# An expert matrix of the slots fetched earlier, in eight blocks of unused rows, and the combine weights turned ahead of the slots' fold

## What is computed

```python
def _moe2_ref(x, phi, w1, w2) -> np.ndarray:
    ...
    logits = x @ phi
    d = logits - logits.max(0, keepdims=True)
    d = np.exp(d)
    d /= d.sum(0, keepdims=True) + 1e-09
    slot_input = d.T @ x
    ...
    for e in range(E):
        h = np.maximum(slot_input[e] @ w1[e], 0.0)
        slot_out[e] = h @ w2[e]
    slot_out = slot_out.reshape(n_slots, D)
    c = logits - logits.max(1, keepdims=True)
    c = np.exp(c)
    c /= c.sum(1, keepdims=True) + 1e-09
    return (c @ slot_out).astype(np.float32)
```

## Time and profile before

| | us |
|---|---|
| median of 3 runs | 384.02 |
| lowest and highest of them | 383.75, 384.81 |
| profiled execution, its own time | 383.24 |
| span of the profiled execution | 381.3 |

### The profile page before, as it was taken

One profiled execution on the slowest core, in us unless ns is written; L12 is line 12 of the kernel. 1 busy time (PEld: TensorE's weight loads), 2 busy tenths in 40 slices (PEclk: granted clock), 3 DMA queues, 4 the chain that ended last, 5 costly groups with the idle time before them and its releaser, 6 DMA issues.

```text
span 381.3 us, 14796 instructions
## 1 busy us (share of the span) xinstructions
PE 352.3 (92%) x5876; PEld 270.6 (71%) x5876; DVE 281.1 (74%) x561; ACT 220.8 (58%) x679; POOL 115.7 (30%) x179
## 2 busy tenths in 40 slices
PE   7699899998999999989999999999999999999780
PEld 7487777777777788666777777777777777664260
DVE  7999999999999744695676777767767767630272
ACT  3777788787888774234656565565656566401051
POOL 3443322334222350064233333222333331651000
PEclk9989999999999999989999999999999999999967
DMA  8987655667657997003085599494949679699539
GB/s 306 412 328 253 257 204 206 238 261 256 234 199 217 402 409 300 21 13 124 22 305 233 189 338 373 170 408 135 391 155 366 213 268 375 229 353 382 194 136 359
DMA packets 31235, 97.58 MB, mean 256 GB/s; under 512 B 3998, under 2 KB 14346, under 8 KB 29658
## 3 DMA queue, kind: packets, MB, share of 16 engines
q1 hardware_dynamic: 29402, 93.81, 66.2%
q0 software_dynamic: 1792, 3.17, 2.7%
HBM read 85.53 MB, written 11.45 MB: 254 GB/s over the span
## 4 chain that ended last, share of the span: by engine, by line
PE 48%; DMA 8%; DVE 8%; issue 1%; ACT 1%; DVEq 0%; SPq 0%; POOLq 0%
PE a_bank L750 19%; PE y_bank L759 18%; DMA combs<-free_rows,put_i 5%; DMA x_all<-combs 2%; PE a_bank L615 2%; PE a_bank L810 1%; PE y_bank L576 1%; PE y_bank L571 1%; DVE x_all L1517 1%; PE a_bank L954 1%; PE ktok_bank L623 1%; PE sums_bank L623 1%; PE y_bank L583 1%; DVE batch_t L1328 1%; DVE free_rows L1501 1%
## 5 line engine op out<-in xcount | busy, mean ns | idle before, releaser
L759 PE MATMUL y_bank<-w_sb,work 128*32 128x192 f32 x1664 | 78.6, 326 | 0.4 <-ACT work L1103 0.4
L750 PE MATMUL a_bank<-w_sb,work 128*32 128x256 f32 x1248 | 77.9, 382 | 0.1
L759 PEld LDWEIGHTS y_bank<-w_sb,work 128*32 128x32 f32 x1664 | 65.3, 110 | 8.2 <-DVE work L1367 0.8
L1553 POOL TENSOR_SCALAR_AFFINE_SELECT a_sb<-a_sb 128x512 f32<-128x512 f32 x48 | 43.2, 911 | 87.3 <-ACT a_sb L988 87.3
L750 PEld LDWEIGHTS a_bank<-w_sb,work 128*32 128x32 f32 x1248 | 42.3, 109 | 25.7 <-issue 13.2
L1076 ACT ACTIVATE work<-work 32x96 f32<-32x96 f32 x108 | 30.4, 282 | 41.4 <-PE a_bank L750 39.1
L998 ACT ACTIVATE bonus_v<-v_sb,bonus 128x48 f32<-128x48 f32 x192 | 45.1, 321 | 14.0 <-DVE x_all L1231 13.9
L1411 DVE TENSOR_TENSOR ys<-work 32x192 f32<-32x192 f32 x104 | 36.3, 349 | 9.9 <-ACT work L1103 9.2
L1367 DVE STREAM_TRANSPOSE work<-hid 128x256 f32<-128x256 f32 x53 | 23.6, 445 | 25.3 <-PE y_bank L759 23.3
L550 PE MATMUL a_bank<-r_in,k_in 64*128 64x128 f32 x384 | 31.1, 297 | 0.1
L550 PEld LDWEIGHTS a_bank<-r_in,k_in 64*128 64x128 f32 x384 | 24.9, 194 | 6.3 <-issue 5.3
(11 more groups left out here) (310 smaller groups left out, 580.0 us busy)
## 6 DMA issues: line engine op xcount, KB each, us to landing
w_sb<-in_moe_w SPq DMA_DIRECT2D x20, 1536.0 KB, 8.2
e_sb<-in_moe_w SPq DMA_DIRECT2D x9, 1536.0 KB, 11.8
wrk_sb<-in_wrk SPq DMA_DIRECT2D x16, 768.0 KB, 7.3
wrk_sb<-in_wrk SPq DMA_DIRECT2D x15, 780.0 KB
v_sb<-in_vt SPq DMA_DIRECT2D x16, 288.0 KB, 2.8
tokens<-x_all SPq DMA_DIRECT2D x4, 1152.0 KB, 22.1
x_all<-in_moe_w SPq DMA_DIRECT2D x3, 1536.0 KB, 9.2
out<-x_all SPq DMA_DIRECT2D x12, 384.0 KB, 3.9
```

The lines of the kernel that those rows point to most:

```text
L750: last = nc.tensor.matmul(out[SUB * g:SUB * (g + 1), 0:FB], x[:, kk, :], w1_sb[j][:, kk, FB * g:FB * (g + 1)], start=(kk == 0), stop=(kk = ...
L759: last = nc.tensor.matmul(bank[4][SUB * g:SUB * (g + 1), 0:YW], h_t[:, SUB * k:SUB * (k + 1)], w2_sb[j][:, k, d:d + YW], start=(b == 0), s ...
L1553: nc.gpsimd.affine_select(out=x, in_=x, compare_op=ALU.is_gt, fill=0.0, base=0, pattern=[[0, 2], [0, 2], [1, C]], channel_multiplier=-1).t ...
```

## The change

It has four parts. First, e2[4] no longer takes blocks 0 to 7 of `x_all` but the eight blocks 14, 15, 16, 25, 26, 27, 28 and 0, in three transfers of 3, 4 and 1 blocks, which SyncE issues right behind e1[5], after `stage_ready` 1. They lie in rows that the 13 groups don't use. Second, e1[7] moves to blocks 1 to 8 and is issued at `slot_parts_full` 2. Third, since `dispatch` still reads the blocks that are being filled, TensorE waits within it: for the first three blocks ahead of group 13, and for all of e2[4] ahead of group 24. The table `combs[3]` is gathered into `disp` and no longer into blocks 25 and 26. Fourth, at the end TensorE turns the combine weights ahead of the fold, ScalarE copies them ahead of its half of `slot_rows`, and VectorE adds the last table ahead of `parts` and makes the norms ahead of its half of `slot_rows`. Two products of the identity that nobody reads follow the fold.

```diff
-                     for t in (logit_t[:, 0:NB, :], weigh_t[:, 0:NB, :], x_all[:, TILES - 3:TILES - 1, :])]
+                     for t in (logit_t[:, 0:NB, :], weigh_t[:, 0:NB, :])] + [disp[:, 0:NT, :]]
...
-        LAST_GROUPS = LAST_PLACE // DM - 2
+        BLOCKS = [14, 15, 16, 25, 26, 27, 28, 0]
+        LAST_GROUPS = BLOCKS[0] - 1
...
-                 7: matrix(x_place[:, WIDE:2 * WIDE], DK, F)}
-        late2 = {4: matrix(x_place[:, 0:WIDE], FK, DM)}
+                 7: matrix(x_place[:, DM:DM + WIDE], DK, F)}
+        late2 = {}
...
+        def e2_rows(e, k):
+            return x_all[:, BLOCKS[k], :] if e == 4 else e2_place(e)[:, k, :]
...
+        def load_e2_blocks(eng, k0, k1, landed):
+
+            eng.dma_start(x_all[:, BLOCKS[k0]:BLOCKS[k0] + k1 - k0, :],
+                          e2[4].rearrange("(k p) d -> p k d", p=P)[:, k0:k1, :]).then_inc(landed, 16)
...
             load_e1(sp, 5)
+            sp.wait_ge(ld_e2[0], 16)
+            sp.wait_ge(stage_ready, 1)
+            load_e2_blocks(sp, 0, 3, ld_e1[5 % EH])
+            load_e2_blocks(sp, 3, 7, ld_e2[0])
+            load_e2_blocks(sp, 7, 8, ld_e2[0])
             sp.wait_ge(slot_parts_full, 2)
-            load_e2(sp, 4)
-            sp.wait_ge(slot_parts_full, 3)
             load_e1(sp, 7)
...
-            dispatch(B1, 4 * BATCH, B1, MAX_GROUPS, x_sorted, bank[1])
+            dispatch(B1, LAST_GROUPS, B1, MAX_GROUPS, x_sorted, bank[1])
             pe.wait_ge(ld_e1[5 % EH], last_landed)
+            dispatch(LAST_GROUPS, 4 * BATCH, B1, MAX_GROUPS, x_sorted, bank[1])
             pe.wait_ge(disp_ready, 5)
-            dispatch(4 * BATCH, MAX_GROUPS, B1, MAX_GROUPS, x_sorted, bank[1])
+            dispatch(4 * BATCH, MAX_GROUPS - 2, B1, MAX_GROUPS, x_sorted, bank[1])
+            pe.wait_ge(ld_e2[0], last_landed)
+            dispatch(MAX_GROUPS - 2, MAX_GROUPS, B1, MAX_GROUPS, x_sorted, bank[1])
...
-            pe.wait_ge(parts_ready, 2)
-            nc.tensor.matmul(bank[3][:, 0:DM // 2], all_parts, parts[:, 0:DM // 2], start=True, stop=True).then_inc(fold_done, 1)
-            nc.tensor.matmul(bank[1][:, 0:DM // 2], all_parts, parts[:, DM // 2:DM], start=True, stop=True).then_inc(fold_done, 1)
             pe.wait_ge(combs_added, 3)
             turn(exps, comb_transposed, 0, 4, bank[6])
             pe.wait_ge(combs_added, 4)
             turn(exps, comb_transposed, 4, NB, bank[7])
+            pe.wait_ge(parts_ready, 2)
+            nc.tensor.matmul(bank[3][:, 0:DM // 2], all_parts, parts[:, 0:DM // 2], start=True, stop=True).then_inc(fold_done, 1)
+            nc.tensor.matmul(bank[1][:, 0:DM // 2], all_parts, parts[:, DM // 2:DM], start=True, stop=True).then_inc(fold_done, 1)
+            idle_products(2, bank[4][:, 0:P])
...
-            dve.wait_ge(slot_back_done, E)
-            V.tensor_scalar(parts[:, 0:DM], bank[2][:, 0:DM], slot_norm[:, :], None, ALU.mult).then_inc(parts_ready, 1)
-            dve.wait_ge(fold_done, 2)
-            V.tensor_copy(slot_rows[:, DM // 2:], bank[1][:, 0:DM // 2]).then_inc(slot_out_ready, 1)
             dve.wait_ge(ld_comb, 16)
             for ns in halves:
                 V.tensor_tensor(comb[:, ns, :], comb[:, ns, :], comb_more[0][:, ns, :], ALU.add).then_inc(combs_added, 1)
+            dve.wait_ge(slot_back_done, E)
+            V.tensor_scalar(parts[:, 0:DM], bank[2][:, 0:DM], slot_norm[:, :], None, ALU.mult).then_inc(parts_ready, 1)
```

More of the change, by code:

```diff
@@ L743, in _ @@
             pe.wait_ge(counts_ready, 3)
-            last_landed = pe.value_load(tiles_i[0:1, E + 5:E + 6], min_val=16, max_val=32)
+            last_landed = pe.value_load(tiles_i[0:1, E + 5:E + 6], min_val=16, max_val=48)
             def first_layer(j, x, out):
@@ L896, in slot_hidden @@
             def slot_hidden(e):
-                pe.wait_ge(ld_e1[e % EH], 16 * (e // EH + 1))
+                pe.wait_ge(ld_e1[e % EH], 48 if e == 5 else 16 * (e // EH + 1))
                 for kk in range(DK):
@@ L913, in slot_back @@
                 h_m = h_early[:, e, :, :] if e < 6 else h_late[:, e - 6, :, :]
-                pe.wait_ge(ld_e2[e % EH], 16 * (e // EH + 1))
+                pe.wait_ge(ld_e2[e % EH], 48 if e == 4 else 16 * (e // EH + 1))
                 for b in range(N // P):
@@ L917, in slot_back @@
                         last = nc.tensor.matmul(bank[2][NS * g:NS * (g + 1), 0:DM], h_m[:, b, NS * g:NS * (g + 1)],
-                                                e2_place(e)[:, g * (N // P) + b, :], start=(e == 0 and b == 0),
+                                                e2_rows(e, g * (N // P) + b), start=(e == 0 and b == 0),
                                                 stop=(e == E - 1 and b == N // P - 1), tile_position=(0, NS * g),
@@ L1162, in _ @@
             nc.scalar.activation(late_own, turned_hidden[:, 6:, :, :], ACT.Copy).then_inc(slot_hidden_t_late, 1)
-            act.wait_ge(fold_done, 1)
-            nc.scalar.activation(slot_rows[:, 0:DM // 2], bank[3][:, 0:DM // 2], ACT.Copy).then_inc(slot_out_ready, 1)
             act.wait_ge(comb_transposed, 1)
@@ L1169, in _ @@
                                  ACT.Copy).then_inc(comb_t_ready, 1)
+            act.wait_ge(fold_done, 1)
+            nc.scalar.activation(slot_rows[:, 0:DM // 2], bank[3][:, 0:DM // 2], ACT.Copy).then_inc(slot_out_ready, 1)
             act.wait_ge(row_norm_ready, 1)
@@ L1513, in _ @@
             V.reciprocal(norm[:, :], norm[:, :]).then_inc(row_norm_ready, 1)
+            dve.wait_ge(fold_done, 2)
+            V.tensor_copy(slot_rows[:, DM // 2:], bank[1][:, 0:DM // 2]).then_inc(slot_out_ready, 1)
             dve.wait_ge(row_norm_ready, 1)
@@ L1601, in _ @@
             nc.gpsimd.tensor_scalar(tiles_i[:, E + 4:E + 5], batches_up[:, 2:3], 1.0, 1.0, ALU.mult, ALU.add)
-            nc.gpsimd.tensor_scalar(tiles_i[:, E + 5:E + 6], batches_up[:, 2:3], -8.0, 32.0, ALU.mult, ALU.add).then_inc(counts_ready, 1)
+            nc.gpsimd.tensor_scalar(tiles_i[:, E + 5:E + 6], batches_up[:, 2:3], -16.0, 48.0, ALU.mult, ALU.add).then_inc(counts_ready, 1)
             pool.wait_ge(x_stored, 16 * B)
```

## The result

The changed kernel takes 381.85 us (median of 4 runs, 381.27 to 382.22). The kernel before, beside it on the same chip, takes 384.27 (4 runs, 383.75 to 384.81). The ratio is 0.9936, with an interval from 0.9922 to 0.995: 2.4 us faster.

What follows compares the result with a forecast made beforehand. The end was taken as bound by full output stores behind a chain of waits from the late gather. Terms of -0.4, -1.1 and 0 gave -1.5 us, so the median goes from 384.02 to 382.5 us; range 381.2 to 383.9.

Steps and rivals of the forecast that it cites:

- Term 1: Gather of `combs[3]` that VectorE awaits: lands at 358.0 and not 358.42, -0.4 us, most freed DMA time returning as idle.
- a transfer flows at once: Rival at the gather: freed DMA time is handed on, landing -1.8 us, time 381.1 us; chance 0.08.
- little comes of it: Rival: the fetch gains 0, the clock falls before the turns so the new order gains 0.5; 383.5 us, chance 0.18.
- term 2: New order at the end: gather's landing to first final product takes 5.70 us and not 6.79, -1.1 us; lower bound 0.5.
- Term 3: Waits inside `dispatch`: 0 us, since e2[4]'s last block lands 1.1 us before TensorE needs it.
- I keep that, because TensorE was at half clock there: First final product to first store: stays at 2.46 us, with TensorE again at half clock.
- the clock stays up: Rival at the final products: full clock makes the first output tile ready 0.7 us sooner; 381.8 us, chance 0.16.
- The clock at its full level at the first product: Sign at TensorE's first final product that, if seen in the changed profile, would make the forecast wrong.
- a fixed 13.6 us: Output stores at the end: DMA stays full, so the time ends 13.6 us behind the first store, unchanged.

Runs made afterwards that it cites:

- c1_after: The changed kernel unchanged, run again in the third set of runs: 388.88 us, ratio 0.9868 to the kernel before.
- The late fetch: Changed kernel with e2[4]'s three transfers issued at `slot_parts_full` 2, as before the change, and e1[7] right behind: 383.61 us, ratio 1.0.
- e1_fetch_only: Changed kernel with the old order put back at the end and no idle products, keeping the early fetch: 383.9 us, ratio 1.0.
- e2_order_only: Changed kernel with loads, places and `dispatch` waits put back as before, keeping the new end order and idle products: 382.24 us, ratio 0.9952.
- c2_order_only: Third-set repeat of the changed kernel with loads, places and `dispatch` waits put back, keeping the new end order: 391.98 us, ratio 0.9955.

## Why the prediction was right, and where it was off

**Term 1, the fetch: right.** -0.4 forecast, -0.39 measured, by the mechanism that was told: the issue of e2[5] stays, and the idle stretch comes back behind e1[7] (335.7 to 340.5 forecast, with the 1.25 us 337.0 to 341.8; read: 336.8 to 341.8). It holds over the other traces too: from the issue of e2[5] to the landing it takes 19.2 to 19.5 us in the eight traces that have the changed kernel's loads, and 19.8 to 20.1 in the three that have the loads of before. Where the landing in the table is late (22.67 in c1_after), e2[5] was issued late (3.43 behind the landmark and not 1.56). The rival that a transfer flows at once is out, and "little comes of it" was not what happened in this trace: term 2 is 1.57 here, though only 0.6 in the trace of c1_after, where the clock fell (6.79 less 6.20). Here are the microseconds behind the issue at 339.77:

```profile
340.00:341.00 1.00, 1.00 (x24) 0.61 (x20) 1.00 (x1) 0.00 (x0) 0.69 (x2) 1.00 0.17 31
341.00:342.00 1.00, 1.00 (x25) 0.62 (x20) 0.27 (x3) 0.00 (x0) 0.83 (x1) 1.00 0.71 120
342.00:343.00 1.00, 1.00 (x27) 0.57 (x23) 0.00 (x0) 0.00 (x0) 0.86 (x1) 1.00 0.98 311
```

The stream is full only 2 us behind the issue, as with e1[7] before. By the trace's single packets the first 1.0 us passes with none (the first one of e2[5] starts at 340.80), and in the second they are still few. The Trainium skill, "DMA: Bandwidth & Descriptors" (Anatomy of one DMA), which has its figures from transfers that GpSimd issues, puts most of the fixed cost of a transfer at its completion. For these transfers of SyncE out of an empty queue the rows, at 339.77, 341.36 and 345.58 alike, show some 2 us ahead of the full stream as well, and the measurement decides.

**Term 2, the new order: the right mechanism, mis-sized by 0.5.** Forecast 5.70 us from landing to product, measured 5.22. The last table, the turns, `parts`, the fold and the norm come in the order that was told, and VectorE's copy ends the wait. I had laid VectorE's steps end to end. Its timeline:

```profile
362.21 0.61 DVE L1523 TENSOR_SCALAR parts<-a_bank,slot_norm 128x384 f32<-128x384 f32 x1
362.74 0.94 DVE L1525 TENSOR_REDUCE norm<-weights_of 128x24 f32<-128x768 f32 x1
...
363.93 0.30 DVE L1527 RECIPROCAL norm<-norm 128x24 f32<-128x24 f32 x1
364.15 0.29 DVE L1529 COPY ys<-a_bank 128x192 f32<-128x192 f32 x1
```

`parts` starts 0.1 ahead of the sum's end (361.27 + 1.03), the reduce 0.08 ahead of the end of `parts`, the copy 0.08 ahead of the reciprocal's end, and it takes 0.29 and not 0.36. That makes the copy end 5.16 behind the landing and not 5.56, and the product follows it by 0.06 and not 0.14. 0.40 and 0.08 are the 0.48.

**Term 3, no wait in** `dispatch`: **right, with less to spare.** TensorE doesn't wait. The last block landed 10.5 us behind its issue at 324.6, at 335.1, and the 17th product starts at about 335.8: 0.7 us of margin where I had 1.1. The late fetch showed that a wait there is handed on to the landmark in full.

**The rest of the sum: the step that failed** is "I keep that, because TensorE was at half clock there". The first store came 1.75 behind the first product and not 2.46, 0.7 us sooner, exactly what the rival "the clock stays up" set. Its time, 381.8, is what came out, to 0.05 us. That closeness is luck: term 2 gained 0.48 more than that rival had it, the way from the first store to the end took 0.38 more, and the two nearly cancel. The clock at its full level at the first product was also one of the signs by which the prediction would call its forecast wrong, and it showed. I had read the clock as a property of the order. The traces say otherwise: with the old order it fell once ahead of the turns (before) and once within them (e1_fetch_only); with the new order it fell within the fold in e2_order_only and in the first turns in c1_after, and stayed full in the other trace of each of these same two kernels. The Trainium skill, "TensorE: Matmul & The Clock Gate" (Part 1), says of the rise of the clock at the start of a kernel that its place varies from run to run. These pairs of traces show the same of its fall. How many executions of the changed kernel keep it stays open, since only profiled ones show it; the case should have had a chance near that of the forecast and not 0.16.

**The stores: not** "a fixed 13.6 us". The stream of the stores itself is the same: in both traces below the window from 0 to 1 us behind the first store moves 71 GB/s, the next eleven 397, the next 280, and then there is nothing. That window from 12 to 13 us, of the changed kernel:

```profile
378.25:379.25 1.00, 0.00 (x0) 0.00 (x0) 0.00 (x0) 0.00 (x0) 0.00 (x0) 0.50 0.72 280
```

and of e2_order_only, which has the loads of before:

```profile
379.29:380.29 1.00, 0.00 (x0) 0.00 (x0) 0.00 (x0) 0.00 (x0) 0.00 (x0) 0.50 0.72 280
```

Yet from the first store to the end it takes 14.00 and 13.62. The difference lies behind the last landing of a store, which comes 13.23 us behind the first store in both traces. SyncE's closing wait passes at 13.25 in both; its next recorded instruction, the drain ahead of the end, starts 0.15 later in e2_order_only and 0.47 later in the changed kernel. It goes with the loads and not with the order or the clock: 13.62 to 13.64 in the three traces with e2[4] in one transfer, 13.99 to 14.01 in the eight with three, 14.26 to 14.27 in the three that split e2[5] too. In these last three it is another thing: one completion of a store comes at 13.87, 0.55 behind all others, and the drain 0.16 behind it as in the kernel before. So the kernel with the early fetch pays back at the very end most of what it wins at the gather, and it can't be seen in the first set when it stands alone. Whether the number of transfers is the cause was not tried and stays open; that SyncE's program has grown by the same edits is a rival.

## What to carry to other kernels

Filling an idle stretch of a stream moves the end only if the next transfer's issue moves too: look first at what releases that issue. Lay a new order out on the engine that is last in it, and treat the clock of a lightly used stretch as a chance and not as a property of the code. The same two kernels can stand 0.4 us apart in one set of runs and 3.1 in another, so try such a part more than once, and find in the trace where the difference lies before you name its cause.

## What was not expected

The kernel before took 384.1 us in the first set and 393.5 and 393.8 in the others, and the changed kernel 381.9 and 388.9. The kernel before has no trace from there; the traces of the other kernels agree with those of the first set up to about 329 us, and then show the stalls that c2_order_only showed above: 3 to 7 us on VectorE, ScalarE and TensorE where the loop of the routed layer ends, and half clock behind them: `dispatch` takes 5.25 us in c2_order_only and 3.42 in the changed kernel. No row names the releaser ("issue" and "remote"), and the packets of the instruction queues weren't visibly longer. That the engines wait there for their next instructions is a guess, and it stays open.
